# A fused attention and two-layer network kernel: the values product of two heads, from two half-width stationary tiles to full-width zero-padded ones

## What is computed

```python
scores = (q @ k.T) / sqrt(64)                 # per batch and head
keep   = (key < 4) | ((0 <= query - key) & (query - key < 128))
a      = softmax(where(keep, scores, -1e9))
x      = (a @ v) -> (1536 tokens, 512)
h = x @ w_in      # 512 x 2048
g = where(h >= 1, h, where(h <= -1, 0, (h + 1)**2 / 4));  x = g @ w_out
h = x @ w_in2
g = where(h > 0, h, exp(min(h, 0)) - 1);                  y = g @ w_out2
```

## Time and profile before

| | us |
|---|---|
| median of three executions | 677.39 |
| lowest, highest | 677.34, 678.03 |
| the profiled execution | 678.03 |
| its span, first to last instruction | 676.2 |
| PE matmul busy | 652.0 |
| PE weight load busy | 629.2 |
| DVE busy | 406.4 |
| ACT busy | 388.5 |

### The profile page before, as it was taken

The page is one execution under the profiler, slowest core; times in us unless marked ns, Lnnn a source line. Parts: engine busy times, 40 slices in busy tenths (PEclk is TensorE's granted clock), DMA queues, the critical chain, the costliest instruction groups (busy, mean ns, idle before and its releaser), DMA issues.

```text
span 676.2 us, 15326 instructions
## 1 busy us (share of the span) xinstructions
PE 652.0 (96%) x5356; PEld 629.2 (93%) x5356; DVE 406.4 (60%) x1130; ACT 388.5 (57%) x1010; POOL 9.5 (1%) x28
## 2 busy tenths in 40 slices
PE   4889999999999999999999999999999999999997
PEld 3668899999999999999999999999999999999997
DVE  6989977886887688678857863333332333323332
ACT  6786765675666667557656664444544544544543
POOL 3000000000000000000000000000000000000000
PEclk9999999999999999999999999999999999999999
DMA  8477221221332033123154400000000000000000
GB/s 268 139 237 275 73 63 48 77 86 38 84 92 67 24 98 84 37 61 88 34 187 156 157 1 2 1 31 0 30 1 0 31 0 0 31 0 0 31 0 31
DMA packets 27340, 45.03 MB, mean 67 GB/s; under 512 B 2929, under 2 KB 17073, under 8 KB 27313
## 3 DMA queue, kind: packets, MB, share of 16 engines
q1 hardware_dynamic: 27312, 44.67, 21.1%
HBM read 41.52 MB, written 3.15 MB: 66 GB/s over the span
## 4 chain that ended last, share of the span: by engine, by line
PE 86%; DVE 9%; ACT 1%; issue 1%; DMA 1%; SPq 0%; ACTq 0%; DVEq 0%
PE y_ps L460 13%; PE h_ps L447 13%; PE y_ps L461 13%; PE y_ps L462 13%; PE h_ps L449 12%; PE h_ps L448 12%; PE o_ps L427 3%; PE t_ps L404 2%; DVE wout_lo L724 1%; PE s_ps L392 1%; PE s_ps L393 1%; DVE win_lo L724 1%; DVE s_ps L678 1%; PE o_ps L433 1%; DVE g_full L744 1%
## 5 line engine op out<-in xcount | busy, mean ns | idle before, releaser
L447 PE MATMUL h_ps<-x_hi,win_hi 128*128 128x256 f32 x768 | 220.4, 287 | 1.8 <-DVE x_lo L730 1.4
L460 PE MATMUL y_ps<-g_hi,wout_hi 128*128 128x256 f32 x768 | 218.1, 284 | 1.1 <-DVE g_lo L735 1.1
L461 PE MATMUL y_ps<-g_lo,wout_hi 128*128 128x256 f32 x768 | 217.3, 283 | 0.0
L462 PE MATMUL y_ps<-g_hi,wout_lo 128*128 128x256 f32 x768 | 217.1, 283 | 0.0
L449 PE MATMUL h_ps<-x_hi,win_lo 128*128 128x256 f32 x768 | 217.0, 283 | 0.0
L448 PE MATMUL h_ps<-x_lo,win_hi 128*128 128x256 f32 x768 | 216.9, 282 | 0.0
L447 PEld LDWEIGHTS h_ps<-x_hi,win_hi 128*128 128x128 f32 x768 | 146.7, 191 | 4.5 <-DVE x_lo L730 1.6
L460 PEld LDWEIGHTS y_ps<-g_hi,wout_hi 128*128 128x128 f32 x768 | 147.3, 192 | 2.9 <-issue 1.4
L462 PEld LDWEIGHTS y_ps<-g_hi,wout_lo 128*128 128x128 f32 x768 | 147.3, 192 | 0.0
L461 PEld LDWEIGHTS y_ps<-g_lo,wout_hi 128*128 128x128 f32 x768 | 147.3, 192 | 0.0
L448 PEld LDWEIGHTS h_ps<-x_lo,win_hi 128*128 128x128 f32 x768 | 146.9, 191 | 0.0
(11 more groups left out here) (114 smaller groups left out, 630.4 us busy)
## 6 DMA issues: line engine op xcount, KB each, us to landing
ks<-in_k SPq DMA_DIRECT2D x44, 260.0 KB, 2.6
qs<-in_q SPq DMA_DIRECT2D x44, 128.0 KB, 2.5
vals<-in_v SPq DMA_DIRECT2D x24, 192.0 KB
raw<-in_w_in SPq DMA_DIRECT2D x6, 512.0 KB, 4.3
raw<-in_w_out SPq DMA_DIRECT2D x6, 512.0 KB, 4.2
out_y<-xy SPq DMA_DIRECT2D x12, 256.0 KB, 2.2
xy<-in_w_in SPq DMA_DIRECT2D x5, 512.0 KB, 5.8
xy<-in_w_out SPq DMA_DIRECT2D x5, 512.0 KB, 6.5
```

Source lines behind the costliest of these rows:

```text
L447: pe.matmul(o, win_hi[:, k, f], x_hi[:, k, :], start=(k == 0), stop=False)
L460: pe.matmul(o, wout_hi[:, t, cols], g_hi[:, t % GR, :], start=(t == 0 and m % 2 == 0), stop=False, skip_group_check=True)
L461: pe.matmul(o, wout_hi[:, t, cols], g_lo[:, t % GR, :], start=False, stop=False, skip_group_check=True)
L462: last = pe.matmul(o, wout_lo[:, t, cols], g_hi[:, t % GR, :], start=False, stop=(t == FT - 1), skip_group_check=True)
```

## The change

`vs` gets its own tile of 192 columns a block: head 0's 64 dimensions, 64 zeros, head 1's 64 dimensions. The stationary factor of a head is now a window of 128 columns, [v0, 0] for head 0 and [0, v1] for head 1, and every matmul writes all 128 partitions, adding zeros on the other head's half. The order is by head and then by block; only head 0's first one starts the accumulation. The host lays the zeros out, so a pair's load is 288 KB in place of 192 KB. The sinks' tile is separate; the lent buffer is a slice of the larger `vs`.

```diff
-        vals = sb("vals", [P, 4 * 2 * P])
-        vs = vals[:, 0:6 * P].rearrange("p (s b d) -> p s b d", s=2, b=3)
-        vsink = vals[:, 6 * P:8 * P].rearrange("p (s d) -> p s d", s=2)
+        vs = sb("vs", [P, 2, 3, 3 * HD])
+        vsink = sb("vsink", [P, 2, P])
...
-                     vals[:, 0:size],
+                     vs[:, :, :, :].rearrange("p s b d -> p (s b d)")[:, 0:size],
...
-                for block, queries, keys_t in ((1, slice(0, CT), slice(P, P + CT)), (0, slice(0, P), slice(0, P)),
-                                               (2, slice(P, CT), slice(P + CT, 2 * CT))):
-                    for hh in halves:
-                        dims = slice(HD * hh, HD * (hh + 1))
-                        pe.matmul(o_bank[dims, queries], vs[:, s, block, dims], probs_t[hh][:, keys_t],
-                                  start=(block == 1), stop=False, skip_group_check=True)
+                for hh in halves:
+                    v, pt = vs[:, s, :, HD * hh:HD * hh + P], probs_t[hh]
+                    pe.matmul(o_bank[:, 0:CT], v[:, 1, :], pt[:, P:P + CT], start=(hh == 0), stop=False, skip_group_check=True)
+                    pe.matmul(o_bank[:, 0:P], v[:, 0, :], pt[:, 0:P], start=False, stop=False, skip_group_check=True)
+                    pe.matmul(o_bank[:, P:CT], v[:, 2, :], pt[:, P + CT:P + CT + P], start=False, stop=False, skip_group_check=True)
...
-    v_w = np.empty((NC, PAIRS, P, 3, 2 * HD), v.dtype)
+    v_w = np.zeros((NC, PAIRS, P, 3, 3 * HD), v.dtype)
...
-            v_w[c, :, :, :, hh * HD:(hh + 1) * HD] = rows[:, hh].transpose(0, 2, 1, 3)
+            v_w[c, :, :, :, 2 * hh * HD:(2 * hh + 1) * HD] = rows[:, hh].transpose(0, 2, 1, 3)
```

## The result

The changed kernel takes 687.40 us (median of four executions, 686.68 to 688.28), the kernel before in the same sessions 677.69: a ratio of 1.0141, 95% interval 1.0127 to 1.0155, +9.7 us. It is slower, as forecast (688.0, +10.6 against the earlier median of 677.39; the kernel before stands 0.3 higher here, so the forecast time is only 0.6 off where the forecast difference is 0.9 off). The profiled execution's span is 685.2 us, 9.0 more than before.

A forecast was written before the change was run, and what follows sets the result against it. PE was taken as the bound beside the layers, except where DVE sets the pace (45 to 87 us). 18 x 0.61 = 10.9, less 0.3 in chunk 0, gave +10.6 us: 688.0 us forecast, range 685.0 to 691.0.

The forecast's parts named there:

- The two heads stream side by side, and lose it: Values product on PE: 12 passes run as 6 doubles, 0.86 us a pair; at full width all 12 run in a row.
- The two gaps go: PE around a pair's values: 0.14 us lost before and 0.20 after, from switching half-width and full-width tiles, both removed.
- Rival 2: PE around the values: plain float32 beside float32r also empties the array; 0.39 more a pair, 695.2 us; 7%.
- A pair costs +0.61: PE, a pair beside a layer: 2.06 us against 1.45, with 128-column passes at 0.12 each.
- rival 1: Values' 128-column passes: the weight load hides, 0.109 a pass; 18 x 0.52 = 9.4, less 0.3: 686.5 us; 13%.
- 18 pairs pay, two are covered: Of 20 pairs beside a layer, PE idle time covers chunk 0's first two; the others add 10.9 us.
- The waits at the chunk's end move along: PE's outward(15) waits for g_lo behind ACT's copy L539; all move 0.61 us later, so the wait absorbs nothing.
- Rival 3: Waits at five chunk ends (0.2 to 0.5 us each) give way, or chunk 0's gain doubles: 2 us less, 686.0; 10%.
- Chunk 0, -0.3: Chunk 0's attention: two one-head calls on the chain gain 0.2 us each, the last pair's 0.8 shows as 0.1.
- Loads: Each pair's load grows by 96 KB, 24 times; at most 1.1 us later against 1.2 us of room: just hidden.
- rival 5: Values' two heads are only recorded together and really ran in turn, so no change in time; 2%.
- Rival 4: Values passes: full width cheaper than half width, a pair 1.15 us, 0.30 less; 5.4 us faster, 671.7; 3%.

The follow-up runs named there:

- the two orders at half width: Kernel before, half-width values reordered: by whole heads, 686.17 us against 678.03; two blocks of a head at a time, 677.96 against 677.72.
- the sinks' halves: Changed kernel with the sinks' product beside a layer cut into two matmuls of 128 columns: 688.34 us, one execution (kernel before 677.72).
- the last two kernels: Half width with padded load, full width only beside chunk 0's layer in pairs 0 and 1: 677.69 us; in pairs 2 and 3: 678.24 (before: 677.72).

## Why the prediction was right, and where its terms were off

- **What bounds it: right.** The kernel grew where PE was the bound, and nowhere else.
- **The two heads stream side by side, and lose it: right**, shown by the timeline and by the two orders at half width. The loss is of the overlap, not of width as such: half-width tiles in an order that keeps the heads apart lose nearly as much (+8.1 us).
- **The two gaps go: right.** Rival 2 (the number type empties the array) falls: L424 is plain float32 between float32r and starts 0.12 behind L460; L431 behind it has no gap either (0.11 for the last L426 and 0.12 for L431 are all that lies between 103.89 and 104.13). In chunk 0, where the sinks' product has 8 rows, the gap is still there in the changed kernel, although both sides are plain float32:

```profile
27.81 0.39 PE L426 MATMUL y_ps<-g_full,vs 128*128 128x128 f32 x2
28.13 0.48 PE L431 MATMUL y_ps<-xy,vsink 8*128 8x256 f32 x1
```

  The last L426 starts at 27.92 and streams till 28.03; L431 starts at 28.13. So the gap follows the size of the tile and not the number type. The Trainium skill, TensorEngine Tiling (Array Packing), Key Properties, says that a change of tiling mode drains the engine, and this agrees with it; the measured price is 0.09 to 0.10 us and the next weight load uncovered. One small tile is an exception: the sinks' transposes have a stationary tile of 8 columns, and the kernel before shows no gap ahead of them (57.80 + 4 x 0.109 = 58.23):

```profile
57.80 0.60 PE L404 MATMUL t_ps<-ident,probs 128*128 128x128 f32 x4
58.23 0.38 PE L410 MATMUL o_ps<-ident,probs 128*8 128x128 f32 x2
```

- **A pair costs +0.61: mis-sized.** It measured +0.54. The step was "behind a float32r-like load, a 128-column pass takes 0.12". Such passes take 0.111 (8 x 0.009 = 0.07 is the difference), although their load lasts 193 ns as predicted: the load's kind was right, and the price that I had tied to it belongs to passes that also stream 256 columns. So rival 1, given 13%, had the mechanism: the load hides but for 0.002 a pass, and the 18 pairs cost 9.7, near its 9.4 and not the 10.9 of the sum. The Trainium skill's load rule (TensorE: Matmul & The Clock Gate, LDWEIGHTS: 107 ns for 128 columns) agrees with the 0.107 to 0.11 of the sinks' halves, if the load is what bounds them. The estimate from it (9.5 in the prediction; its own terms, 18 x 0.52, give 9.4) was the better one.
- **18 pairs pay, two are covered: right**, by the steps and by the last two kernels. **The waits at the chunk's end move along: right.** Rival 3's first half falls. A chunk grew by 2.2, inside the stated 2 to 3, and no new wait of PE appeared.
- **Chunk 0, -0.3: not shown.** In the changed kernel's profiled execution ACT casts `win_hi` 0.70 earlier (37.50; 38.20 before), yet the first layer's first matmul starts 0.20 later than before (38.56 and 38.36), since the last pair of chunk 0 takes 0.9 longer up to L431's second pass (36.01 to 38.25; before 36.71 to 38.05), near the 0.8 that I had:

```profile
37.50 1.04 ACT L563 CAST win_hi<-raw 128x1024 fp32r<-128x1024 f32 x1
38.56 0.38 PE L445 MATMUL h_ps<-x_hi,win_hi 128*128 128x256 f32 x1
```

  PE then waits less for `x_lo`, and from 45 us on the execution is 0.7 us ahead, twice what I had. But kernels whose chunk 0 has half-width tiles start the first layer anywhere from 37.50 us (pairs 2 and 3 at full width) to 38.63 (full width beside the layers only), and 38.36 in the kernel before. The spread is larger than the gain, and the medians with and without the full-width calls agree within 0.15%. The sum (10.9 - 0.3 = 10.6) came near 9.7 with one term 1.2 too high and one of which nothing can be seen; that this second term lay on the right side was luck as far as the runs show.
- **Loads: right.** The padded load costs nothing.
- **Rivals 4 and 5** fall with the timeline, rival 5 also with the half-width order by heads, where the overlap is lost and the time rises. Rival 4's price was misread besides: it takes 0.06 for the transposes' pace, and the earlier trace rows show 0.109.

## What to carry to other kernels

Before small tiles are padded to full width, look at whether two starts stand together in the timeline: the pair then pays for one, and doubling the passes must be weighed against a gap of 0.09 us and an uncovered load at each switch. Put the passes of different tiles close together in the order, though they need not alternate strictly (here two products of one half could stand in front of the other's, three could not). Price a pass by the distance between starts of passes that have both its load and its number of columns, and count only the places where that engine is the bound.

## What the runs showed of the hardware

- Passes of one half of the array went ahead of three earlier ones of the other half, which had not started (0.48 us lost a pair with six in front, none with four).
- Float32r passes with 128 stationary columns step by 0.107 to 0.11 us for 128 columns and by 0.12 for 256. Float32 passes of 128 columns step by 0.109 with 64 stationary columns and by 0.109 to 0.112 with 128, so there the longer load adds next to nothing. The transposes step by 0.109 with 128 stationary columns and with 8 alike, so the load doesn't set their pace.
- TensorE's clock can drop for a moment in chunk 0's first layer steps. In the kernel with pairs 0 and 1 at full width, PE was busy 0.72 of 2.00 us before 41 us, and the next 3 us ran at 1.2 GHz, half of 2.4; the kernel before was busy 0.69 of the same 2.00 and stayed at 2.4. In the kernel with the padded load alone the mean of the same 3 us was 0.60 of 2.4. The drop was not free. The kernel with pairs 2 and 3 at full width is, up to pair 0's values, the same program as the one with pairs 0 and 1, and it stayed at 2.4. The two stood 0.06 us apart at their first layer matmul (37.56 and 37.50) and 0.52 apart at the same matmul some 14 us later (51.98 and 51.45), by the low clock or what came with it. Columns as in the earlier trace rows; the clock is the third number from the end:

```profile
39.00:41.00 2.00, 0.72 (x4) 0.72 (x5) 1.99 (x4) 1.06 (x3) 0.00 (x0) 0.89 0.61 153
41.00:44.00 3.00, 3.00 (x16) 3.00 (x15) 2.57 (x5) 2.14 (x4) 0.00 (x0) 0.50 1.02 361
44.00:48.00 4.00, 4.00 (x36) 4.00 (x35) 3.81 (x10) 3.52 (x7) 0.00 (x0) 1.00 0.66 250
```
